# Attention, cosine-gated layer and routed experts on one core: scores by row halves, the top-32 mask as a penalty under the exponential, fractions on GpSimd

## The reference

```
q, k, v: (2 batches, 8 heads, 576 positions, 64)
scores = q @ k.T / 8
kth    = the 32nd largest score of each row
attn   = exp(scores - max) where scores >= kth, else 0
attn   = attn / (sum(attn) + 1e-9)
x      = attn @ v               # (1152, 512), rows = batch * position
h = x @ w_in                    # (1152, 2048)
g = h * cos(h)
y = g @ w_out                   # (1152, 512)
```

## Time and profile before

| | |
|---|---|
| median of 3 runs | 705.64 us (704.75, 705.64, 706.73) |
| span of the profiled execution, first to last instruction | 704.2 us |
| its mean granted TensorE clock | 0.963 |
| TensorE, VectorE, ScalarE, GpSimd busy | 91%, 79%, 55%, 53% |

### The profile page before, as it was taken

How to read it: one execution, slowest core, us unless ns; L and a number is a source line. 1 busy time by engine, 2 the same in 40 slices (tenths; PEclk the granted TensorE clock), 3 DMA queues, 4 the chain that set the end, 5 groups by cost and what they waited for, 6 DMA issues and landing times.

```text
span 704.2 us, 12713 instructions
## 1 busy us (share of the span) xinstructions
PE 639.4 (91%) x4148; PEld 540.1 (77%) x4148; DVE 558.0 (79%) x1009; ACT 388.3 (55%) x603; POOL 372.5 (53%) x278
## 2 busy tenths in 40 slices
PE   5577998999999999999999999989719999999996
PEld 2455876987887887887988988879619887888884
DVE  3999999989799799899898898424536677776673
ACT  2444675575575485575675673733506555566450
POOL 0669997488587588587597685850340111001111
PEclk9787999999999999999999999999958999999999
DMA  9697000000000000000000000032159445675510
GB/s 347 267 354 282 10 10 15 24 9 15 22 15 9 24 17 9 30 9 7 30 7 27 3 0 16 1 124 101 61 211 375 161 184 239 261 279 220 188 50 14
DMA packets 17642, 70.89 MB, mean 101 GB/s; under 512 B 1982, under 2 KB 6590, under 8 KB 15040
## 3 DMA queue, kind: packets, MB, share of 16 engines
q1 hardware_dynamic: 15856, 65.63, 24.4%
q0 software_dynamic: 1744, 4.73, 2.0%
HBM read 56.69 MB, written 14.45 MB: 101 GB/s over the span
## 4 chain that ended last, share of the span: by engine, by line
PE 58%; DVE 17%; issue 9%; POOL 6%; DMA 5%; ACT 4%; DVEq 0%; POOLq 0%; SPq 0%; ACTq 0%
DVE top L354 7%; DVE arena L357 6%; PE p_o L1058 5%; PE p_a L1095 5%; PE p_b L1095 4%; PE p_b L1121 4%; PE p_t L1040 3%; PE p_b L1123 3%; PE p_b L1122 3%; DMA wff<-slot_rows 2%; PE p_s L1023 2%; PE p_s L1025 2%; PE p_o L1282 2%; PE p_o L1284 2%; PE p_o L1283 2%
## 5 line engine op out<-in xcount | busy, mean ns | idle before, releaser
L354 DVE MAX8 top<-arena 128x8 f32<-128x576 f32 x288 | 203.4, 746 | 22.3 <-ACT arena L750 22.3
L357 DVE MATCH_REPLACE8 arena<-top,arena 128x576 f32<-128x576 f32 x216 | 158.6, 741 | 0.0
L612 POOL TENSOR_SCALAR mask<-arena,top 128x576 f32<-128x576 f32 x72 | 127.4, 1769 | 30.2 <-DVE top L354 23.6
L616 POOL TENSOR_TENSOR arena<-arena,mask 128x576 f32<-128x576 f32 x72 | 103.5, 1437 | 30.4 <-ACT arena L764 20.0
L1058 PEld LDWEIGHTS p_o<-arena,probsT 128*128 128x128 f32 x640 | 82.8, 200 | 8.7 <-ACT probsT L771 5.5
L1058 PE MATMUL p_o<-arena,probsT 128*128 128x65 f32 x640 | 83.5, 280 | 3.9 <-ACT probsT L771 3.9
L771 ACT COPY probsT<-p_t 128x640 f32<-128x640 f32 x72 | 50.0, 695 | 65.2 <-PE p_t L1040 65.2
L750 ACT COPY arena<-p_s 128x576 f32<-128x576 f32 x72 | 46.0, 639 | 53.1 <-PE p_s L1024 27.9
L1040 PEld LDWEIGHTS p_t<-ident,arena 128*128 128x128 f32 x360 | 44.1, 148 | 36.1 <-POOL arena L616 25.4
L1121 PE MATMUL p_b<-w_out_lo,g_hi 128*128 128x512 f32 x144 | 62.1, 431 | 6.7 <-DVE g_lo L397 6.7
L1040 PE MATMUL p_t<-ident,arena 128*128 128x128 f32 x360 | 54.8, 285 | 13.5 <-POOL arena L616 13.4
(11 more groups left out here) (168 smaller groups left out, 1352.0 us busy)
## 6 DMA issues: line engine op xcount, KB each, us to landing
arena<-in_w SPq DMA_DIRECT2D x8, 2048.0 KB, 8.9
wff<-in_w SPq DMA_DIRECT2D x8, 2048.0 KB, 9.2
slot_rows<-y_now SPq DMA_DIRECT2D x1, 4626.0 KB, 25.9
q_sb<-in_qpad SPq DMA_DIRECT2D x36, 128.0 KB, 2.4
wff<-in_w_out SPq DMA_DIRECT2D x1, 4096.0 KB, 21.3
wff<-in_w_in SPq DMA_DIRECT2D x1, 4096.0 KB, 14.2
wff<-slot_rows SPq DMA_DIRECT2D x8, 385.5 KB, 3.9
arena<-in_vones SPq DMA_DIRECT2D x2, 1300.0 KB, 10.9
```

Of the source, the lines that this page charges most:

```text
L354: nc.vector.max(best, src).then_inc(top_step, 1)
L357: nc.vector.match_replace(work[:, a, :], best, src, LOWEST).then_inc(top_step, 1)
L612: nc.gpsimd.tensor_scalar(mask[:], s_sb[:, t, :], top[:, t, TOP_K - 1:TOP_K], None, ALU.is_ge).then_inc(mask_made, 1)
L616: nc.gpsimd.tensor_tensor(probs[:, t % 2, :], probs[:, t % 2, :], mask[:], ALU.mult).then_inc(probs_ready, 1)
```

## The change

- **Scores by row halves.** Two heads of one batch now share the partitions: even heads on 0 to 63, odd heads on 64 to 127. `q_sb` and each batch's `kT` have half the size, and the keys of batch 1 come in a transfer of their own behind w_out. A pair's scores are four matmuls, even, odd, even, odd, each with 64 contracted rows, and the last of them waits on a semaphore for the first, because both write the middle bank. Block 4 splits each into two of 64 queries.
- **Order.** A pair's scores stand at odd t, ahead of that head's transpose: t = 1 pair 3 of the block, t = 3, 5, 7 pairs 0, 1, 2 of the next.
- **Mask as a penalty.** GpSimd makes `biases` from the largest and the 32nd value (times -1/8, and times 2^80). ScalarE makes `pen` = relu(2^80 * kth - 2^80 * score), which is 0 for the top 32 (`pens`). GpSimd subtracts it from `s_sb` in place. ScalarE takes the exponential of that into `probs`. The comparison and the multiplication on GpSimd are gone.
- **Fractions.** All four quarters are made by GpSimd, in `odd_whole`; VectorE makes them only for the last block.
- ScalarE's and GpSimd's orders change with that.

```diff
-SPOT = [0, 3 * 512 - S]
-LAG = 4
+SPOT = [288 + 512, 512 - 288]
+SPLIT = [512 - 288, 288]
+WHOLE = slice(0, P)
+FIRST_KEYS, LATER_KEYS = [(WHOLE, 0)], [(WHOLE, 1)]
+MIXED_KEYS = [(slice(0, D), 0), (slice(D, P), 1)]
+AHEAD = 3
...
         @block.vector
...
-                    fraction(i - 2, 3, 2 * (i - 2) + 2, odd_turns_ready)
...
-                    fraction(i - 1, 1, 2 * (i - 1) + 1, odd_turns_ready)
...
         @block.gpsimd
...
+            def bias(i, p):
+
+                wait(pool, top_step, 56 * i + 14 * p + 14)
+
+                wait(pool, probs_ready, 8 * i + 2 * p - 6)
+                nc.gpsimd.tensor_tensor(biases[:, 2 * p:2 * p + 2, :], top[:, 2 * p:2 * p + 2, 0:TOP_K:TOP_K - 1],
+                                        signs[:].unsqueeze(1).broadcast_to([P, 2, 2]),
+                                        ALU.mult).then_inc(biases_ready, 1)
+
+            def mask_tile(i, t):
+                wait(pool, pen_ready, 8 * i + t + 1)
+                nc.gpsimd.tensor_tensor(s_sb[:, t, :], s_sb[:, t, :], pen[:, t % 2, :],
+                                        ALU.subtract).then_inc(masked, 1)
...
+                bias(i, 1)
                 masks(i, 1)
                 if first:
                     low_w_out(0)
                 if second:
                     low_w_out(4)
                     low_w_out(5)
+                bias(i, 2)
                 if up:
                     fraction(i - 1, 0)
-                masks(i, 2, 2 * (i - 1) + 1 if up else None)
+                masks(i, 2)
                 if first:
                     low_w_out(1)
                 if up:
-                    gated(i - 1, 0)
-                mask_tile(i, 6)
-                if up:
-                    fraction(i - 1, 2)
-                mask_tile(i, 7, 2 * (i - 1) + 2 if up else None)
+                    fraction(i - 1, 1)
+                bias(i, 3)
+                masks(i, 3)
                 if first:
                     low_w_out(2)
                 if up:
-                    gated(i - 1, 1)
+                    gated(i - 1, 0)
+                    fraction(i - 1, 2)
+                if more:
+                    bias(i + 1, 0)
+                if up:
+                    fraction(i - 1, 3)
                 if more:
                     masks(i + 1, 0)
-
+                if up:
+                    gated(i - 1, 1)
...
         @block.scalar
...
+            def pens(i, p):
+
+                wait(act, biases_ready, 4 * i + p + 1)
+                for t in (2 * p, 2 * p + 1):
+                    wait(act, masked, 8 * i + t - 1)
+                    nc.scalar.activation(pen[:, t % 2, :], s_sb[:, t, :], ACT.Relu, bias=biases[:, t, 1:2],
+                                         scale=-FAR).then_inc(pen_ready, 1)
+
+            def exps(i, p):
+                for t in (2 * p, 2 * p + 1):
+                    wait(act, masked, 8 * i + t + 1)
+
+                    wait(act, pT_ready, 8 * i + t - 1)
+                    nc.scalar.activation(probs[:, t % 2, :], s_sb[:, t, :], ACT.Exp, bias=biases[:, t, 0:1],
+                                         scale=SCALE).then_inc(probs_ready, 1)
...
         @block.tensor
...
+                piece_of(0, 0, SPLIT[0]).then_inc(middle_bank_done, 1)
+                piece_of(1, 0, SPLIT[1])
+                piece_of(0, SPLIT[0], S)
+
+                wait(pe, middle_bank_done, 4 * blk + p + 1)
+                piece_of(1, SPLIT[1], S).then_inc(scores_done, 2)
```

More of the change, by code:

```diff
@@ L831, in body @@
             def body(i, up=True, down=True, mixed=False, batch=0, more=True):
-                scores(i, 4)
+                first, second = not up, up and not down
                 copy_pT(i, 0)
-                scores(i, 5)
-                if up and not down:
+                pens(i, 1)
+                if second:
                     high_w_out(4)
+                scores(i, 3)
                 copy_pT(i, 1)
@@ L857, in body @@
                     copy_h(i - 1, 0)
+                pens(i, 2)
+                if more:
+                    scores(i + 1, 0)
                 copy_pT(i, 3)
@@ L871, in body @@
                     cosine(i - 1, 0)
-                exps(i, 3, both=False)
-                exp_tile(i, 6)
-                if not up:
+                if first:
                     high_w_out(1)
+                pens(i, 3)
+                if more:
+                    scores(i + 1, 1)
                 copy_pT(i, 5)
@@ L896, in body @@
                     cosine(i - 1, 1)
+                if more:
+                    pens(i + 1, 0)
+                    scores(i + 1, 2)
                 copy_pT(i, 7)
@@ L903, in body @@
                 copy_o(i, 1)
-            for t in range(LAG):
-                scores(0, t)
+            for p in range(AHEAD):
+                scores(0, p)
+            pens(0, 0)
             exps(0, 0)
@@ L1150, in gate, with body @@
                 last.then_inc(logits_ready, 1)
-            def body(i, up=True, down=True, mixed=False, batch=0, more=True):
+            def body(i, keys, next_keys, up=True, down=True, mixed=False, batch=0, more=True):
                 def part(t, half):
@@ L1187, in body @@
                     part(t, 1)
[L1188 to L1190 removed]
             pe.wait_ge(const_step, NCONST)
[L1193 to L1196 removed]
+            for p in range(AHEAD):
+                scores(0, p, FIRST_KEYS)
+            body(0, FIRST_KEYS, FIRST_KEYS, up=False, down=False)
+            body(1, FIRST_KEYS, FIRST_KEYS, down=False)
+            with pe.Fori(2, MIXED - 1) as i:
+                body(i, FIRST_KEYS, FIRST_KEYS)
+            body(MIXED - 1, FIRST_KEYS, MIXED_KEYS)
+            body(MIXED, MIXED_KEYS, LATER_KEYS, mixed=True)
+            with pe.Fori(MIXED + 1, NBLK - 1) as i:
+                body(i, LATER_KEYS, LATER_KEYS, batch=1)
+            body(NBLK - 1, LATER_KEYS, None, batch=1, more=False)
             last_blk = NBLK - 1
```

193 lines of the change are left out of this document (77 added, 116 removed).

## The result

The kernel takes 728.58 us after the change (median of four runs, 722.85 to 729.30) against 705.91 before (four runs on the same chip, 704.75 to 706.73). The ratio is 1.0307, with a 95% interval of 1.0279 to 1.0335: slower, by about 22 us. The prediction was 728 with a range of 714 to 749. The profiled execution took 728.42 around a span of 726.7, 22.5 more than before, at a mean granted clock of 0.947 (0.963 before).

The account below looks back on a forecast made before the run. TensorE paced before; now the ring would, at 53.7 us a block. Span 704.2 plus 21.5 (-1, +2.0, -5.6, +22.2, +3.9) gives 725.7, 727 as the runs' median, 728 with g_lo interference; range 714 to 749.

Parts of the forecast that it names:

- the ring: Up-projection, copy, fraction, cosine, gate, g_hi, g_lo, down-projection: forecast to take 53.7 us a block against 46.6 of TensorE work.
- D: Mark on TensorE: start of the third quarter of down_half; a wait of about 2.3 us was forecast in front of it.
- U: Mark on TensorE: end of the first quarter of up_half; from there to D was forecast at 38.2 us against 34.5.
- U of block 1 to D: First ring, from 83.10 to the end of g_lo: 36.2 us becomes 38.2, so +2.0.
- seven D to U and six U to D: Steady blocks: 7 x -0.8 = -5.6 from shorter scores, 6 x 3.7 = +22.2 from the longer ring.
- U of block 8 to the last `g_hi`: Block 8, with no next pair: 31.0 us where it was 27.1, so +3.9.
- row halves don't overlap: Rival on TensorE's scores: 1.0 us a block more between D and U and some at U, +8, 736; chance 12%.
- The walk: Step-by-step timing from U = 0 through ScalarE, GpSimd and VectorE to D at 38.2 us, +3.7 against 34.5.
- Two masks and their penalty now stand between cosine 1 and its gate: Main cause between U and D: before, the gate came first; 3.6 us.
- Fraction 1 waits, fraction 3 begins behind fraction 2: Other main causes: fraction 1 waits on GpSimd for masks and the copy, fraction 3 for fraction 2; 2.90 us a fraction.
- The table load before the Relu: Rival on ScalarE: each penalty's Relu needs a table load on the ring, 15 x 1.28 = 19, 747; chance 10%.
- The clock as a rival: Rival: clock falls in new waits, 4.3 us of work behind the wait at D at half speed, +30, 758; chance 4%.

Follow-up runs that it names:

- extra matmuls: The changed kernel with five matmuls into unused columns in front of TensorE's wait at t = 6; 714.98 us, ratio 1.0156.
- both gates first: The changed kernel with extra matmuls and GpSimd's two gates ahead of the masks before them, each g_hi moved earlier on ScalarE; 710.30 us (721.27 without the matmuls).
- all of it: The changed kernel with both gates ahead of the masks, fractions 1 and 3 on VectorE with the table load ahead of the wait, and extra matmuls; 706.07 us.
- the new order of the halves: The changed kernel with a pair's score pieces programmed even, even, odd, odd; the trace showed the old order; 727.85 us.
- the second wait: The changed kernel with a second, long-met wait (on h's copy) before each sine; the table load still ran first; 727.29 us.
- the VectorE experiment: The changed kernel with fractions 1 and 3 back on VectorE and two waits before the sine; 729.74 us, ratio 1.0337.

## Why the prediction was right

The sign, the size and the place were right: the ring through `g_lo` paces the block, and TensorE waits in front of D. The total is within 1 us. That is partly the luck of terms that cancel. The terms against the two traces (the first two columns are changes against before):

| term | predicted | measured |
|---|---|---|
| start to U of block 1 | -1 | -0.3 (83.10 to 82.80) |
| U of block 1 to D | +2.0 | +1.9 (38.2 after) |
| seven D to U and six U to D | +16.6 | +19.6 (D 120.98 to U 461.30, before 119.37 to 440.12) |
| U of block 8 to the last `g_hi` | +3.9 | +1.6 (461.30 to 490.01) |
| the rest | 0 | -0.3 |
| span | +21.5 | +22.5 |

- **Scores.** Predicted 1.3 us a pair within 1.05 and 2.3, measured 1.44 at full clock: the halves overlap, not fully. The Trainium skill, TensorEngine Tiling (Array Packing), section Theoretical Speedup, gives up to twice the speed for a dimension of 64, an estimate of 1.05; no run here comes to it. D to U was put at 15.5 and is 15.7 to 15.8. The rival "row halves don't overlap" falls, and the halves alone gain 1.3% (11 us).
- **The walk, step by step**, from U at 296.58: the copy of quarter 0 ends at 1.2 (predicted 1.27), fraction 0 at 4.4 (4.47), the masks at 7.1 (7.3), the copy of quarter 1 at 9.2 (9.4), fraction 1 at 12.4 (12.55). Then the first error: the sine ends at 13.4, not 15.0. I put the table load of 1.28 behind the wait; it ran ahead of it, at both sines. The earlier trace rows show no wait there, but the other cosine of the same block before the change has the load behind a wait for VectorE's fraction:

```profile
311.44 1.28 ACT L796 ACT_TABLE_LOAD   x1 [0.20 <-DVE turns L378]
```

  The kernel before has two waits in front of the sine, the change one. The prediction took the load's old place for the new one.
- **Masks and gate** keep their length but that lead: gate 0 ends at 19.5 (21.1), gate 1 at 33.6 (35.75). The biases cost 1.19 once instead of 0.2, beside VectorE's `g_lo`, which took 2.21 there.
- **The end of the walk failed in the other direction.** `g_hi` should have begun at 35.8, at the gate's end. The gate ended at 33.6, and `g_hi` began at 36.7, behind the copy of the scores, which TensorE had made at half clock. Without the fall of the clock U to D is 36.1 (extra matmuls), against 34.5 before and 38.2 predicted. So the two errors, 2.1 too much by the load and the gate's end and 3.1 too little by the clock, leave 39.2 in a steady block and 38.4 in the mean of the six.
- **Named causes.** "Two masks and their penalty now stand between cosine 1 and its gate" is true of the list, but taking it away gains nothing on its own once the clock is full (51.8 against 51.9), since `g_hi`, put ahead of ScalarE's copies, hands its wait on to `probsT`. "Fraction 1 waits, fraction 3 begins behind fraction 2": moving them gains 0.4 a block at most. With the clock held by the extra matmuls, both gates first take 4.7 us off in all (714.98 to 710.30), the fractions 2.4 (712.56), and all of them 8.9 (706.07).
- **Waits.** Predicted 7.1 us a block on TensorE; the rows have 2.29 + 1.74 = 4.0, because the work at half clock fills the other 3. The wait for `probsT` in the steady block isn't there.
- **The rivals.** The table load before the Relu isn't there: the Relu (323.94) follows the sine (322.97) at once. The Trainium skill, ScalarE: Activation LUTs, section Table sets, has relu in every set; the trace agrees. The clock as a rival had 4%, at D, at 30 us. It came at t = 6, the wait that I had priced but not asked the same question of, and costs 13.6 us.
- **The factor for VectorE.** The fractions took 2.9 us each on GpSimd as priced (298.05 to 300.95). The estimate by the Trainium skill, GPSIMD Engine Reference, section Key points (VectorE about twice as fast for elementwise work), was 16 us less; the rows make it 2.5 times for a fraction (2.90 against 1.15, with three instructions against two).

What stays open: why the clock falls behind some waits of 2.3 to 2.5 us and not behind others of the same length (by the Trainium skill, TensorE: Matmul & The Clock Gate, Part 1, the monitor that gates the clock runs free of the kernel, so that the same wait can be met at another moment of it; no run here shows this); what the "all of it" kernel does without its extra matmuls; and what the penalty costs by itself, since no experiment kept the old mask within the new orders. The version to keep is the kernel before with the row halves alone.

## What to carry to other kernels

When a ring paces a kernel, walk it through the in-order queue of each engine that it passes: the instruction that ends the ring may be ready early and stand behind one that depends on another part of the ring. Ask of every new wait on TensorE, not only the longest, what the work behind it costs at the lower clock level. Time a change of several parts part by part: here the first part gains 11 us and the others lose 34. And look in the trace whether an experiment's edit did what it was made for: here the new order of the halves and the second wait did not.

## What the runs showed of the hardware

- TensorE's granted clock fell from 1.00 to 0.50 behind a single wait of 2.29 us and came back about 7 us later; another kernel's wait of 2.28 us at the same step (366.19) had full speed behind it. About 2.4 us of matmuls without a use, in front of the wait, kept the clock and made the kernel 13.6 us faster.
- ScalarE's table load of 1.28 us ran ahead of the unmet wait of its sine where that wait was the only one (306.36 after the change). With two waits it stood behind the one for VectorE's fraction before the change (311.44) and in the VectorE experiment (365.68), and ahead of the unmet one where the second had long been met (358.00).
- VectorE's `g_lo` and GpSimd's two-input passes get in each other's way. `g_lo` took 2.21 us instead of 1.23 where it overlapped a fraction's last pass for 1.1 us (317.81 to 318.95), and the small product of GpSimd that began beside it took 1.19 instead of 0.20 and ended just behind it (320.09 and 320.02). No run isolated this.
- Two score matmuls in different halves of the rows overlap in part: 1.44 us a pair for 2.11, the first two starting within 0.02 us of each other.
